# Keys and queries transposed raw and placed by transfers, reciprocals spread through DRAM, values kept in one copy

## The reference, cut to what matters

```python
# q, k, v: (4 batches, 8 heads, 1152 positions, 64); factor 2
q_pool = q.reshape(B, H, S // 2, 2, D).mean(axis=3)            # 576 pooled queries a head
scores = scale * np.matmul(q_pool, k.transpose(0, 1, 3, 2))    # 576 x 1152
scores = scores - np.max(scores, axis=-1, keepdims=True)
attn = np.exp(scores)
attn = attn / (np.sum(attn, axis=-1, keepdims=True) + 1e-09)
attn_out = np.matmul(attn, v)                                  # 576 x 64 a head

x = attn_out.transpose(0, 2, 1, 3).reshape(2304, 512)
h = x @ w_in                                                   # 512 -> 2048
x = piecewise_curve(h) @ w_out                                 # clamp, square, max
h = max(x @ w1, x @ w2, x @ w3)                                # 512 -> 768, three gates
out = h @ w2_out
```

## Time and profile before

| | |
|---|---|
| Three runs | 1293.17 us median (1292.42 to 1294.87) |
| The profiled execution | 1294.91 us, its span 1293.0 us |
| PE, PEld busy | 97%, 93% of the span |
| DVE, ACT, POOL busy | 59%, 51%, 26% |
| DMA | 49.07 MB, mean 38 GB/s |

### The profile page before, as it was taken

How to read it: one execution, slowest core, us unless ns; L and a number is a source line. 1 busy time by engine, 2 the same in 40 slices (tenths; PEclk the granted TensorE clock), 3 DMA queues, 4 the chain that set the end, 5 groups by cost and what they waited for, 6 DMA issues and landing times.

```text
span 1293.0 us, 21136 instructions
## 1 busy us (share of the span) xinstructions
PE 1259.6 (97%) x7876; PEld 1207.9 (93%) x7876; DVE 758.1 (59%) x1579; ACT 658.8 (51%) x1570; POOL 335.5 (26%) x332
## 2 busy tenths in 40 slices
PE   7999999999999999989999999999999999999998
PEld 6989899999989898979999999999999999999997
DVE  5888888888888888874544444444453222223221
ACT  5989899999989898962222222222222111111111
POOL 5343443444433444258600000000282000000000
PEclk9999999999999999989999999999999999999999
DMA  3111111111111111113300000000030000000000
GB/s 119 47 56 56 52 33 57 53 41 56 56 47 56 56 56 38 52 49 100 113 1 1 1 1 1 1 1 1 17 122 26 1 25 25 1 25 5 20 25 25
DMA packets 59140, 49.07 MB, mean 38 GB/s; under 512 B 2977, under 2 KB 48033, under 8 KB 59041
## 3 DMA queue, kind: packets, MB, share of 16 engines
q1 hardware_dynamic: 59040, 47.72, 12.1%
HBM read 42.99 MB, written 4.72 MB: 37 GB/s over the span
## 4 chain that ended last, share of the span: by engine, by line
PE 79%; ACT 18%; DVE 1%; issue 1%; POOL 1%; DMA 0%; SPq 0%; POOLq 0%; ACTq 0%
PE hid L868 33%; PE acc L900 16%; ACT probs L558 8%; PE trans L413 8%; ACT pT_hi L548 6%; PE acc L932 6%; PE scores L456 6%; PE values L475 5%; PE scores L458 4%; ACT kT L568 1%; ACT value_aux L582 1%; PE trans L424 1%; DVE qT L662 1%; ACT X L578 1%; ACT qT L571 1%
## 5 line engine op out<-in xcount | busy, mean ns | idle before, releaser
L626 DVE TENSOR_REDUCE neg_max_parts<-scores 128x1 f32<-128x384 f32 x432 | 234.7, 552 | 44.0 <-PE scores L458 30.3
L548 ACT ACTIVATE pT_hi<-trans 128x384 fp32r<-128x384 f32 x432 | 191.2, 491 | 55.8 <-PE trans L413 52.3
L640 DVE TENSOR_TENSOR pT_lo<-trans,pT_hi 128x384 fp32r<-128x384 f32 x432 | 212.0, 546 | 7.3 <-ACT pT_hi L548 6.3
L558 ACT ACTIVATE probs<-scores,neg_max 128x768 f32<-128x768 f32 (+1 forms) x288 | 212.0, 753 | 4.0 <-DVE neg_max L633 4.0
L456 PE MATMUL scores<-kT,qT 128*128 128x384 f32 x480 | 199.6, 416 | 9.4 <-ACT probs L558 9.1
L413 PE MATMUL trans<-ident,probs 128*128 128x128 f32 x1296 | 189.7, 273 | 9.6 <-DVE qT L662 6.4
L413 PEld LDWEIGHTS trans<-ident,probs 128*128 128x128 f32 x1296 | 157.5, 140 | 24.9 <-DVE qT L662 11.5
L868 PE MATMUL hid<-qT,w_slots 128*128 128x384 f32 x936 | 171.6, 336 | 0.0
L868 PE MATMUL hid<-x_hi,w_slots 128*128 128x384 f32 x624 | 167.6, 335 | 0.0
L868 PEld LDWEIGHTS hid<-qT,w_slots 128*128 128x128 f32 x936 | 163.7, 188 | 1.0
L986 ACT ACTIVATE excess<-rise,halves 128x384 f32<-128x384 f32 x96 | 59.2, 617 | 203.0 <-DVE rise L1070 203.0
(11 more groups left out here) (101 smaller groups left out, 1998.2 us busy)
## 6 DMA issues: line engine op xcount, KB each, us to landing
k_raw<-in_k SPq DMA_DIRECT2D x16, 576.0 KB, 4.0
v_raw<-in_v SPq DMA_DIRECT2D x32, 288.0 KB, 2.8
q_raw<-in_q SPq DMA_DIRECT2D x32, 256.0 KB, 3.0
out<-X SPq DMA_DIRECT2D x18, 256.0 KB, 2.8
q_raw<-in_moe_w_out SPq DMA_DIRECT2D x14, 256.0 KB, 3.1
k_raw<-in_moe_w SPq DMA_DIRECT2D x12, 256.0 KB, 3.1
k_raw<-in_moe_w_in SPq DMA_DIRECT2D x8, 256.0 KB, 2.9
k_raw<-in_moe_w_out SPq DMA_DIRECT2D x8, 256.0 KB, 3.0
```

The costliest lines, as they stand in the source:

```text
L548: act.activation(*tile_places(pT[0], src, t, g), ACT.Copy).then_inc(p_hi_done, 1)
L558: act.activation(probs[:, par, :].rearrange("p (n k) -> p n k", n=GROUPS)[:, ns[0]:ns[-1] + 1], scores[:, bank:bank + len(ns), 0:SB], ACT. ...
L626: dve.tensor_reduce(neg_max_parts[:, par, n:n + 1], scores[:, score_banks(u9)[n], 0:SB], AX_X, ALU.max, negate=True).then_inc(parts_done, 1)
L640: dve.tensor_tensor(*tile_places(pT[1], src, t, g), hi.bitcast(F32), ALU.subtract).then_inc(p_lo_done, 1)
```

## The change

1. **Keys.** `k_raw` is laid out with the two heads side by side (pieces of 64 elements, 256 B). PE transposes it unsplit: three groups K0 to K2 of three blocks. ACT writes the high part and DVE the low part to `k_parts` (head 0 on partitions 0 to 63, head 1 on 64 to 127), and four transfers of 64 partitions x 4608 B put the parts where `kT` wants them (`place_k`). The mixed tile multiplies `k_parts` directly: three matmuls a bank.
2. **Queries.** Two heads side by side too: Q0 is four blocks, Q1 the mixed tile alone. ACT and DVE write `q_parts`, eight transfers of 64 partitions x 2048 B make the stacked copies (`place_q`).
3. **Reciprocals** go to a DRAM tensor, element by element (`send_recips`), and come back broadcast over partitions (`spread_recips`). POOL multiplies `X` with them (`scale`). PE's R groups and DVE's `scale_x` are gone.
4. **Values.** ACT copies a product once, all 128 rows, to `value_all`; a transfer moves the other half to `value_aux` (`move_values`); POOL adds.
5. **Orders** are written out lap by lap, all pairs unrolled. Eight weights are split early instead of three, the early hidden products are gone, and `split_x` waits only for the pairs that its tokens need.
6. The first pair keeps the old way (`first_...`), with its keys also copied to `k_parts`.

The new orders, and what SP does for a pair:

```diff
+PE_ORDER = """
+S1.1 T0.0 S1.2 T0.1 T0.2 S2.0 W2:10-18 Q0
+S2.1 T1.0 S2.2 T1.1 T1.2 S3.0 W3:0-8 Q1
+S3.1 T2.0 S3.2 T2.1 T2.2 S4.0 W3:8-13
+S4.1 T3.0 S4.2 T3.1 T3.2 S5.0 W3:13-18 K0
+S5.1 T4.0 S5.2 T4.1 T4.2 S6.0 V0:0-8 K1
+S6.1 T5.0 S6.2 T5.1 T5.2 S7.0 V0:8-18 K2
+S7.1 T6.0 S7.2 T6.1 T6.2 S8.0 V1:0-8
+S8.1 T7.0 S8.2 T7.1 T7.2 S9.0 V1:8-18
+S9.1 T8.0 S9.2 T8.1 T8.2 S10.0 V2:0-10
+"""
...
+        for i in range(PAIRS):
+            if i > 0:
+                send_recips(i - 1)
+            if i + 1 < PAIRS:
+                place_q(i + 1)
+            if i + 2 < PAIRS:
+                sp.wait_ge(q_trans_done, (i + 1) * QG)
+                load_q(i + 2)
             load_v(i, 1)
...
+            if i > 0:
+                move_values(i - 1, 2)
+                spread_recips(i - 1)
+                move_values(i - 1, 3)
+            if i + 1 < PAIRS:
+                load_v(i + 1, 0)
+            if i + 2 < PAIRS:
+                sp.wait_ge(k_trans_done, (i + 1) * KG)
                 load_k(i + 2)
...
+            if i + 1 < PAIRS:
+                place_k(i + 1)
+            else:
+                load_weights(0)
+                load_weights(1)
+            move_values(i, 0)
+            move_values(i, 1)
```

The parts:

```diff
         def load_k(pair):
...
+            for h in range(2):
+                src = k_heads[bass.ds(head(pair) + h, 1)].rearrange("h p (t d) -> p (h t) d", d=D)
+                sp.dma_start(k_raw[:, :, h, :], src).then_inc(k_loaded, 16)
...
+        def place_k(pair):
+
+            sp.wait_ge(k_lo_done, pair * KG)
+            for h in range(2):
+                for a in range(2):
+                    copy_parts(sp, kT[rows_of(a), pair % 2, h, :], k_parts[rows_of(h), a, :], k_placed)
...
+        def send_recips(pair):
+
+            sp.wait_ge(recip_done, pair + 1)
+            sp.dma_start(recip_rows[pair % 2].rearrange("(t p) -> p t", p=P), recips[:],
+                         allow_slow_non_contiguous=True).then_inc(recip_sent, 16)
...
+            if n == 0 and t == 0 and pair > 0:
+                pe.wait_ge(k_placed, 64 * pair)
+                pe.wait_ge(q_placed, 128 * pair)
...
+                pe.matmul(out, hi, k_parts[:, 0, keys], start=True, stop=False)
+                pe.matmul(out, lo, k_parts[:, 0, keys], start=False, stop=False)
+                last = pe.matmul(out, hi, k_parts[:, 1, keys], start=False, stop=True)
...
+        def scale(pair):
+
+            pool.wait_ge(recip_spread, 48 * (pair + 1))
             pool.sem_inc(passed, 1)
...
+            x = X[:, bass.ds(pair * SQ, SQ)]
+            pool.tensor_tensor(x, x, recip_cols[:], ALU.mult).then_inc(scaled, 1)
...
+            act.activation(value_all[:, n % 2, :], values[:, 0:HALF], ACT.Copy).then_inc(value_kept, 1)
...
+            dve.tensor_tensor(k_parts[:, 1, cols], trans[:, BANK["K", pair, g], 0:GK * P],
+                              k_parts[:, 0, cols].bitcast(F32), ALU.subtract).then_inc(k_lo_done, 1)
...
-    EARLY = 3
+    EARLY, EARLY_LOADS = 8, 4
```

More of the change, by code:

```diff
@@ L144, in prep_of, with ring_order @@
[L144 to L149 removed]
+    WARM_UP, BRIDGE = 22, 10
+    FIRST = [("FK", 0), ("FK", 1), ("FK", 2), ("FQ", 0)]
+    SECOND = [("FK", 3), ("FK", 4), ("FK", 5), ("FQ", 1), ("FQ", 2)]
+    def ring_order():
+        groups = FIRST + SECOND
+        for pair in range(PAIRS):
+            for step in steps_of(PE_ORDER):
+                if step[0] == "T":
+                    groups.append(("T", pair * TILES + step[1], step[2]))
+                elif step[0] in "KQ" and pair + 1 < PAIRS:
+                    groups.append((step[0], pair + 1, step[1]))
+        return groups
@@ L467, in value_products @@
+            last.then_inc(scores_done, 1)
+        def value_products(pair, n, products):
+            h, half = n // 2, n % 2
+            t = (2, M_TILE, 7, TILES - 1)[n]
             for m in products:
@@ L942, in two_tiles1 @@
                 for f in range(C1):
-                    if not (first and u == 0 and f < EARLY):
-                        hidden1(pe, tile, f, u)
+                    hidden1(pe, tile, f, u)
                     if f >= LAG1:
```

990 lines of the change are left out of this document (489 added, 501 removed).

## The result

The changed kernel takes 1492.74 us (median of 4 runs, 1490.69 to 1494.65), the kernel before 1293.16: a ratio of 1.154 (95% interval 1.152 to 1.156). The forecast was 1319 us, with a range of 1256 to 1350. Slower was the likelier side and right; the size was missed by 174 us.

A forecast was written before the change was run, and what follows sets the result against it. PE was taken as the first bound, DVE the second. A pair was to go from 35.3 to 37.2 us (30.0 + 0.8 + 4.4 stall + 2.0 clock): 1293.0 + 29 - 5 + 2 = 1319 us, range 1256 to 1350.

The forecast's parts named there:

- Engines, undisturbed pair: Attention pair without transfer stalls: DVE becomes the bound at 32.5 us, 2.8 us less a pair.
- SP issues 30 transfers a pair ... covered as long as its waits come in time: SP's queue in each attention pair: 30 issues instead of 8, 13 us of issuing, hidden.
- the sum: From K2's end on PE to placed keys landing: 9.2 us against 4.75 of PE's work, so a 4.4 us stall.
- The reciprocals ... at a 512 B piece's price they take 2 us, unseen: Send of 1152 4-byte elements to DRAM in each pair: 2 us, hidden.
- rival 4: Reciprocals hold the queue, delaying the queries' placing from 15 us on, 2 us a pair more: 1350 us, chance 0.05.
- The placing's way: Transfers of keys between pairs: load 3.0 us, placing 4.7, start 1.0 and landing 0.5.
- rival 2: Half rate: keys' placing takes 5.8 us, PE stands 5.5, a pair takes 38.8: 1343 us, chance 0.20.
- The Trainium skill's two rules: Keys' transfers: 196 GB/s on 64 partitions (placing 6.0 us); read-modify-write below 512 B (load at 4.0 us or above).
- The clock: PE at half clock after each stall at the next pair's first scores: 2.0 us lost per stall.
- The ends: Attention's end 5 us shorter by adds ahead of splits; start 2 us longer by the first pair's key copy.
- S9.0: Next pair's first scores on PE, reached 4.75 us after K2's end; PE was to stand there 4.4 us.

The follow-up runs named there:

- e5: Changed kernel with reciprocals sent as 128 pieces of 36 B and keys placed only once (later pairs score against old keys): 1284.8 us, 0.994 of before.
- e2: Changed kernel with the next pair's keys placed ahead of the loads of values and keys in SP's order: 1413.2 us, 1.093 of before.
- e1: Changed kernel with reciprocals sent as 128 pieces of 36 B instead of 1152 of 4 B, in wrong order: 1432.7 us, 1.109 of before.
- e4: Changed kernel with keys placed only once, for the second pair, so later pairs score against old keys: 1335.7 us, 1.033 of before.
- e6: Changed kernel with nine groups of transfers ahead of it, each waited for, to time them by themselves: four placing transfers took 5.1 us.
- e3: Changed kernel with both the 36-byte send of reciprocals and the placing of keys ahead of the loads: 1368.1 us, 1.058 of before.
- e15: e10 with first queries transposed one lap later, third key group back in its own lap, keys placed in two groups: 1274.8 us, 0.986 of before.
- e10: e8 with the third key group transposed a lap earlier, no 4-byte send left, first queries transposed as in the changed kernel: 1306.0 us, 1.009 of before.
- e8: Changed kernel made whole: keys placed in three groups ahead of loads, reciprocals sent as rows after PE transposes, last pair's in 4-byte pieces: 1317.1 us, 1.019 of before.
- e9: Changed kernel with POOL's first add of second-head values behind the split of the next values instead of ahead: 1502.1 us, 1.161 of before.
- e17: Changed kernel with transfers ahead of it: a straight copy behind the 4-byte send (send landed after 10.5 us) and behind the 36-byte send (copy through in 3 us).

## Why the prediction was right or wrong

- *Engines, undisturbed pair.* 32.5 us forecast from rows, with bounds of 31.5 and 33.8; the steady pair of e5 takes 33.2, of which DVE, the busiest engine, works for 30.2. Right within the bounds, and DVE with it. What the change can give is 35.0 - 33.2 = 1.8 us a pair, not 2.8: 0.7 is missing because this pair is longer than forecast, and 0.3 because the forecast was held against one of the longer pairs of before.
- *"SP issues 30 transfers a pair ... covered as long as its waits come in time".* This step failed. Its waits didn't: the placing of keys was issued 6.95 us behind K2's low part, where the sum had it at once. The sum took SP's queue as an issuer at 0.45 us a transfer; it is also a line of data in order, and a line of waits for other engines. In the pair shown these are 7 of the 10.8 us by which the keys came later than PE; e2, which takes the load of keys and the wait for POOL's split out of the placing's way, cut the wait for kT from 10.1 to 3.8 us a time. The 13 us of issuing were too few as well: 28 of the 30 issues of that pair took 24 us, and 18 us in the pair of e1.
- *"The reciprocals ... at a 512 B piece's price they take 2 us, unseen".* This failed in size: 10.5 us from issue to landing, and what stood behind it was held. The mechanism was rival 4, at a chance of 0.05, with effect only from 15 us on and 2 us a pair as its price. It is 3.3 us a pair without the placing (e4 against e5) and 3.6 with it (changed against e1), 51 and 60 us in all.
- *The placing's way*: load and placing together were 3.0 + 4.7 us, and 8.0 us from the first placing issue (1.25) to the landing (9.2). Measured: 2.6 + 5.1 by themselves, and 9.3 us in the pair. The placing's 5.1 us are within the bounds, between the forecast's 4.7 and rival 2's 5.8, and e6 shows somewhat over rival 2's half rate (216 and 232 against 401 GB/s). In the kernel the way is longer than its parts: 7.7 us in e3 with no load ahead, where the sum's terms give 0.9 + 4.7 + 0.5 = 6.1.
- *The Trainium skill's two rules.* The four placings alone ran at 232 GB/s of busy time, one at 216. The Trainium skill's page "SBUF — State Buffer" (section Door 1) gives two readings for partitions 0 to 63, 196 GB/s measured at 1 MiB and about 218 as what long transfers approach. The trace, which counts busy time alone, agrees with the second; the estimate of 6.0 us that the prediction drew from the first is 0.9 above the 5.1 measured, and the measurement decides. The load of 256-byte pieces took 2.6 us. By the Trainium skill's page "DMA: Bandwidth & Descriptors" (Specifications), which has read-modify-write below 512 B, the prediction saw it at 4.0 us or above. The trace does not agree with that size, though these pieces did run slower, at 225 GB/s against 300 for those of 512 B. The prediction did not weigh that rule against the 4-byte pieces, which are the ones that cost.
- *The clock.* 2.0 us a stall was forecast. After the stall of 11 us here the clock stays at 0.50 for about 3 us behind it, so that the value products behind it take about double, as in the earlier trace rows. The same nine in the changed kernel and in e5:
```profile
298.08 2.25 PEld L550 LDWEIGHTS values<-pT_lo,v_split 128*128 128x128 f32 x9
291.99 1.24 PEld L550 LDWEIGHTS values<-pT_lo,v_split 128*128 128x128 f32 x9
```
  PEld's whole pair is 30.9 us busy in the changed kernel and 29.5 in e5, so the low clock cost about 1.4 us there, less than forecast. With the stall of 10.8 us this leaves some 3 of the 15 us between the two pairs that no run assigns. Where the stall is gone the low clock is gone: two pairs of e15, by windows,
```profile
300.00:366.00 66.00, 64.01 (x446) 58.13 (x444) 59.32 (x141) 57.07 (x144) 21.15 (x24) 1.00 0.56 135
```
  run at 1.00.
- *The ends.* -5 and +2 were forecast. The gap of the earlier trace rows that the -5 stood for lies in the last distance, and that is 4.1 us shorter, so this step was about right. What the sum lacked stands behind it: +11 at the end, and +12.7 at the start. At the end the adds do stand ahead of the splits, but behind the last 4-byte send in the queue; with that send gone e10 ends 8.4 us sooner than e8. Of the start's 12.7 us 5.7 are the first of the 15 stalls, which the sum had among the pairs, and 4.2 the wait for the first queries, against 2 forecast for all.

The direction was right, for part of the reason: PE does stand at S9.0 for the placing. But a steady pair was forecast at 37.2 us and took about 48, and what is missing is what a queue in order does to the transfers that stand behind slow and waiting ones.

## What to carry to other kernels

Read a DMA queue like an engine in order: for each transfer that somebody waits for, add up what stands ahead of it (issues, data, and SP's own waits on other engines), and move the urgent one ahead of prefetches; this alone gave 80 us here. A transfer of 1152 single 4-byte elements to DRAM costs what stands behind it some 10 us; transpose on PE first and send whole rows. A reordering that shortens one wait is not a gain until the total says so: in e9 58 us left one wait, 45 came back in the next, and the kernel was 9 us slower. And compare a steady pair with a steady pair: the average over all fifteen distances would have made e5 look like the forecast to 0.1 us, where it was 0.7 off.

## What the runs showed of the hardware that was not expected

- 1152 pieces of 4 B from SBUF to DRAM: the packets show 0.5 us of engine time, the transfer lands after 10.5 us, and transfers behind it move at 30 to 50 GB/s for most of that time with a busy share of about 1.0 (48 GB/s over 6 us in e17, 33 and 29 in the changed kernel). A busy share alone says nothing of progress. 128 pieces of 36 B: 1.4 us.
- SBUF to SBUF through 64 partitions on each side: 216 GB/s for one transfer, 232 for four in a row on both halves; 401 through 128.
- 256-byte pieces from DRAM ran at 225 GB/s of busy engines, 512-byte ones at 300.
- SP's issues do not cost the same everywhere: the eight placings of queries took 4.95 us in e1 (0.6 each) and 7.39 behind the 4-byte send (0.9 each), the four placings of keys behind a load 4.8 us in both (1.2 each). That a full queue is the reason is likely, but not shown.
